# The order of TensorE's work within a step of an attention stage: weighing the values ahead of preparing later heads

## The chip, the cores and the metric

One core of a Trainium2 chip. The time is device microseconds (us) of one execution of the whole program. An engine is TensorE (PE; its weight loads are PEld), VectorE (DVE), ScalarE (ACT), GpSimd (POOL) or SyncE (SP, which here only issues DMAs).

## The reference

Attention over 2 batches, 8 heads, 768 positions and 64 columns, in which a query sees only keys of its own cluster (16 a head, the nearest centroid by cosine). Two feed-forward blocks over 1536 tokens follow.

```python
q_assign = np.argmax(np.einsum('bhsd,hcd->bhsc', q_n, c_n), axis=-1)
k_assign = np.argmax(np.einsum('bhsd,hcd->bhsc', k_n, c_n), axis=-1)
mask = q_assign[:, :, :, None] == k_assign[:, :, None, :]
scores = np.where(mask, scale * np.matmul(q, k.transpose(0, 1, 3, 2)), -1000000000.0)
scores = scores - np.max(scores, axis=-1, keepdims=True)
attn = np.exp(scores); attn = attn / (np.sum(attn, axis=-1, keepdims=True) + 1e-09)
x = heads side by side of np.matmul(attn, v)          # 1536 x 512
h = (x @ moe_w1) * (x @ moe_w2) @ moe_w3 @ moe_w_out
h = h @ moe2_w_in; out = (max(h, 0) + alpha * min(h, 0)) @ moe2_w_out
```

## The kernel before, in words

Every fp32 product is made from a rounded high part and a low remainder (names ending in h and l), as two or three fp32r matmuls. The order of work of all engines is written out by hand, step by step, and each engine has its own queue; they meet in semaphores.

The attention stage walks over the 16 heads in steps, one per tile of 128 queries (6 a head, 96 in all). A turn is 4 heads (24 steps): the first 11 steps are a prologue, then a loop and two written-out turns follow. In step c, TensorE's `step` (L667) puts into its queue:

- `score(c)` (L612): four matmuls into one of two PSUM slots. It waits until ScalarE's exponential has read tile c - 2.
- `turn_probabilities(c - 4)` (L631): six transposes of exponentials, three into each bank of `turned_p`, each bank once VectorE has read the low part `pl` of the tile before from it.
- what `prepared` (L54) lists for this step. It repeats every 12 steps: in steps 10, 11, 0 and 1 of the twelve half a head is turned (`turned`, L583: three transposes of q and k side by side into bank 0 of `acc`), in steps 2 and 3 a half of the cluster scores of two heads is made (`cluster`, L598: six matmuls into the same bank). All of these belong to heads that are scored later. Each waits until the bank is read (`prep_free`).
- `weigh(c - 5)` (L649): four matmuls that multiply turned probabilities by v and add them up in bank 1 of `acc` over three tiles. The first of a group of three (c = 2, 5, 8, 11 of the twelve) waits until ScalarE has copied the group before out of the bank (`drained`); the first tile of a head (c = 5 and 11) also waits for GpSimd's splitting of v (`v_done`).

ScalarE's `step` (L932): `out_copy` of a finished group (L921), the two copies `ph` of the turned probabilities (L914), scaling of the turned operands if there are any (`operands_hi`, L899), the exponential of tile c (L906), x's high part (`x_hi`, L927). In steps 2, 5, 8 and 11 the output copy comes first, and in steps 4 and 10 the high part last.

VectorE's `step` (L1163): the maximum of tile c (L1147), `pl` (L1152), then the low part of the operands (`operands_lo`, L1115), or the transposing of the cluster scores (L1123), or a step of picking the clusters (L1132).

GpSimd's `step` (L536): picking (L478), folding and normalising a finished head (L512), splitting v (L465), x's low part (L528). SyncE's `step` (L343) issues the DMAs for it: half a head of x moved to other partitions, copies of the operands that stack high and low parts (`stack_first` L300 behind a turned head, `stack_second` L307 behind the cluster scores), masks, the row of inverses, the next q, k and v.

The last turn prepares nothing. There are 26 turned tiles in steps (steps 0 and 1, then 24) and 14 halves of cluster scores (steps 2 and 3, then 12); the first ones stand in steps c = 0 to 3, where nothing is yet weighed. Behind the attention stage, from about 304 us, the feed-forward blocks run on the same engines.

Of the kernel before, what the change touches and what calls it, by code (L numbers as in the profile page):

```python
# [39 lines left out]
LT, LW, LX = 4, 5, 6  # L40
# [13 lines left out]
def prepared(it, c, last):  # L54

    j, m = c // 12 * 2, c % 12
    plan = {0: [("turned", j + 3, 0)], 1: [("turned", j + 3, 1)], 2: [("cluster", j + 2, 0)], 3: [("cluster", j + 2, 1)],
            4: [("pick1", j + 2, 0)], 6: [("pick2", j + 2, 0)], 9: [("pick3", j + 2, 0)],
            10: [("turned", j + 4, 0)], 11: [("turned", j + 4, 1)]}.get(m, [])
    there = HB if last else 2 * HB if isinstance(it, int) and it == TURNS - 2 else 3 * HB  # L60
    return [(kind, head, half) for kind, head, half in plan if head < there]
# [31 lines left out]
def build(nc, q, k, v, cen, w1, w2, w3, wo, w_in, w_out, alpha, out):  # L93
    ctx = ExitStack()
    with ctx:
# [162 lines left out]
        def tile(it, c):  # L258

            return TILES * it + c  # L260

        def head(it, j):

            return HB * it + j
# [313 lines left out]
        def _(pe):  # L578
            def mm(o, a, b, start, stop):
                return nc.tensor.matmul(o, a, b, start=start, stop=stop)  # L580


            def turned(it, j, half, first=False):  # L583

                f = fill_of(it, "turned", j, half)
                o = acc[:, half if first else 0, :]
                pe.wait_ge(ld_qk[j % 2], 32 * (2 * it + (j // 2 + 1)))
                if not first:
                    pe.wait_ge(prep_free, f)
                elif j > 0:  # L590
                    pe.wait_ge(prep_free, f - 1)
                for t in range(3):
                    last = nc.tensor.transpose(o[:, t * P:(t + 1) * P],
                                               qk[j % 2][:, 3 * half + t, :, :].rearrange("p a d -> p (a d)"),
                                               ident[:, :])
                last.then_inc(prep_full, 1)

            def cluster(it, j, half, first=False):  # L598

                f = fill_of(it, "cluster", j, half)  # L600
                cols, o = slice(half * HS, (half + 1) * HS), acc[:, half if first else 0, 0:HS]
                pe.wait_ge(prep_free, fill_of(it, "cluster", j, 0) if first else f)
                pe.wait_ge(cwin_done, head(it, j + 2))
                for e in range(2):
                    h = (j + e) % HB
                    w = cwin[h][:, :, 64 - 64 * e:192 - 64 * e]
                    mm(o, w[:, 0, :], q1[h][:, cols], e == 0, False)
                    mm(o, w[:, 1, :], q1[h][:, cols], False, False)
                    last = mm(o, w[:, 0, :], k1[h][:, cols], False, e == 1)
                last.then_inc(prep_full, 1)  # L610

            def score(it, c):  # L612


                j, t = divmod(c, T6)
                h, q_tile, o = j % HB, slice(t * P, (t + 1) * P), scores[c % 2]
                if c >= 2:
                    pe.wait_ge(exp_done, tile(it, c - 1))
                elif c == 1:
                    pe.wait_ge(w3_lo, NF)  # L620
                if t == 0:
                    pe.wait_ge(stacked2[h], 32 * (it + (j // HB + 1)))
                    pe.wait_ge(masked[h], 32 * (it + (j // HB + 1)))
                for half in range(2):
                    mm(o[:, half, 0:HS], q1[h][:, q_tile], k1[h][:, half * HS:(half + 1) * HS], True, False)
                for half in range(2):
                    last = mm(o[:, half, 0:HS], q2[h][0:96, q_tile], k2[h][0:96, half * HS:(half + 1) * HS],
                              False, True)
                last.then_inc(score_full, 1)

            def turn_probabilities(it, g):  # L631


                first_tile, a = g // 3 * 3, g % 3
                if a == 0:
                    pe.wait_ge(exp_done, tile(it, first_tile + 3))
                if g == 0:
                    pe.wait_ge(wc_out, NF)
                for b in range(2):
                    if g >= 1:  # L640
                        pe.wait_ge(pl_done, 2 * tile(it, g) + b - 1)
                    key_tile = 2 * a + b
                    for i in range(3):
                        p = pf[(first_tile + i) % NPF][:, :, :].rearrange("p a t -> p (a t)")
                        last = nc.tensor.transpose(turned_p[:, b, i * P:(i + 1) * P],  # L645
                                                   p[:, key_tile * P:(key_tile + 1) * P], ident[:, :])
                    last.then_inc(t_full, 1)

            def weigh(it, g):  # L649


                j, a = g // T6, g % 3
                pe.wait_ge(pl_done, 2 * tile(it, g) + 2)
                if a == 0:
                    if g == 0:
                        pe.wait_ge(prep_free, FILLS + 2)
                    else:
                        pe.wait_ge(drained, 2 * HB * it + g // 3)
                if g % T6 == 0:
                    pe.wait_ge(v_done, head(it, j + 1))  # L660
                for b in range(2):
                    w = v12[j % 2][:, 2 * a + b, :]
                    mm(out_acc, w, ph[g % NPH][:, b, :], a == 0 and b == 0, False)
                    last = mm(out_acc, w, pl[g % NPH][:, b, :], False, a == 2 and b == 1)
                last.then_inc(pv_done, 1)

            def step(it, c, last):  # L667
                there = lambda g: g >= 0 and (not last or g < TILES)
                if there(c):
                    score(it, c)  # L670
                if there(c - LT):
                    turn_probabilities(it, c - LT)
                for kind, j, half in prepared(it, c, last):
                    if kind == "turned":
                        turned(it, j, half)
                    elif kind == "cluster":
                        cluster(it, j, half)
                if there(c - LW):
                    weigh(it, c - LW)


            def turn_w3(f, parity):
# [74 lines left out]
            for c in range(LEAD):  # L757
                step(0, c, False)
                if c < 4:
                    if c % 2 == 0:  # L760
                        pe.wait_ge(wc_out, NF - 3 + c // 2)
                    product_wc(c // 2, range(4 * (c % 2), 4 * (c % 2) + 4))
            with pe.Fori(0, TURNS - 2) as it:
                for c in steps():
                    step(it, c, False)
            for c in steps():
                step(TURNS - 2, c, False)
# [545 lines left out]
```

## Time and profile before

| | |
|---|---|
| time, median of 3 runs | 787.78 us (786.77 to 788.28) |
| the profiled execution's time | 788.31 us |
| its span, first to last instruction | 786.5 us |
| mean granted TensorE clock | 0.993 of full speed |
| busy: TensorE, its weight loads | 762.0 us, 647.5 us |
| busy: VectorE, ScalarE, GpSimd | 418.9, 329.3, 188.1 us |
| attention stage | from about 56 to 304 us |

A row of the profile's groups and of the timeline names the line, the engine, the operation and what it writes and reads. Matmuls overlap, so TensorE's busy time says little about its peak; where a step stands is best read from the start of its weight loads. An idle time is given in brackets with what ended it.

### The profile page before, as it was taken

The numbers are of one execution on the slowest core, as the hardware profiler recorded it, in microseconds if no ns is written. First come the engines' busy times: TensorE is split into PE (matmuls) and PEld (weight loads), VectorE is DVE, ScalarE is ACT, GpSimd is POOL, SyncE is SP. The second block draws the span as 40 slices with busy tenths as digits, with TensorE's granted clock in tenths as the row PEclk, the third lists the DMA queues.
The fourth block names the chain that finished last, engine by engine and source line by source line (L and its number), as shares of the span: only waits on it lengthen the run. The fifth ranks groups of instructions, "written<-read, shape, count | busy, mean of one in ns | idle before, by whom it ended". The sixth has DMA issues, their size and how long they took to land.

```text
span 786.5 us, 10717 instructions
## 1 busy us (share of the span) xinstructions
PE 762.0 (97%) x3810; PEld 647.5 (82%) x3810; DVE 418.9 (53%) x636; ACT 329.3 (42%) x643; POOL 188.1 (24%) x210
## 2 busy tenths in 40 slices
PE   5999999999999998899999999999999999999998
PEld 4888998898899897788888888878888888888886
DVE  5335988989889886443211143276333443333332
ACT  4335978878888885532211142242112101020102
POOL 2131486876876873300000000000000000000000
PEclk9999999999999998999999999999999999999999
DMA  9645455554564322230000021232000000010001
GB/s 295 161 121 127 87 125 132 134 137 114 123 151 106 92 47 74 73 108 1 0 1 1 0 81 54 80 93 69 0 1 23 32 1 1 1 53 1 1 0 54
DMA packets 63579, 54.17 MB, mean 69 GB/s; under 512 B 31264, under 2 KB 51760, under 8 KB 63536
## 3 DMA queue, kind: packets, MB, share of 16 engines
q1 hardware_dynamic: 63536, 53.59, 26.4%
q8 instruction: 28, 0.46, 0.2%
q14 instruction: 15, 0.12, 0.0%
HBM read 31.50 MB, written 3.19 MB: 44 GB/s over the span
## 4 chain that ended last, share of the span: by engine, by line
PE 76%; POOL 15%; issue 5%; DVE 2%; ACT 2%; DMA 1%; POOLq 0%; SPq 0%; ACTq 0%
PE slot L580 55%; PE acc L580 17%; POOL xf L525 3%; PE slot L645 3%; POOL xf L521 2%; POOL xl L531 2%; POOL v L474 1%; POOL oh L500 1%; POOL v L470 1%; POOL c L492 1%; PE slot L693 1%; POOL c L493 1%; POOL c L498 1%; POOL c L490 1%; DMA early<-in_moe_w_out 1%
## 5 line engine op out<-in xcount | busy, mean ns | idle before, releaser
L580 PE MATMUL slot<-xh,w 128*128 128x512 f32 x768 | 252.7, 395 | 0.0
L580 PEld LDWEIGHTS slot<-xh,w 128*128 128x128 f32 x768 | 144.3, 188 | 34.9
L580 PE MATMUL slot<-xl,w 128*128 128x512 f32 x384 | 151.8, 395 | 0.0
L1049 ACT CAST gh<-gf 128x512 fp32r<-128x512 f32 x48 | 29.8, 621 | 207.8 <-PE acc L580 190.4
L1155 DVE TENSOR_TENSOR pl<-slot,ph 128x384 fp32r<-128x384 f32 x192 | 97.7, 549 | 14.0 <-ACT ph L919 13.8
L1149 DVE TENSOR_REDUCE nm<-slot 128x1 f32<-128x768 f32 x96 | 91.2, 950 | 21.4 <-PE slot L580 21.0
L919 ACT CAST ph<-slot 128x384 fp32r<-128x384 f32 x192 | 83.6, 487 | 40.4 <-PE slot L645 39.6
L911 ACT ACTIVATE pf<-slot,nm 128x768 f32<-128x768 f32 x96 | 87.9, 915 | 8.7 <-DVE nm L1149 8.5
L580 PEld LDWEIGHTS slot<-xl,w 128*128 128x128 f32 x384 | 72.2, 188 | 17.2
L645 PE MATMUL slot<-ident,pf 128*128 128x128 f32 x576 | 81.9, 277 | 1.9 <-DVE pl L1155 1.6
L580 PE MATMUL slot<-k,q 96*128 96x384 f32 (+1 forms) x384 | 83.6, 339 | 0.0
L1281 DVE TENSOR_TENSOR gl<-gf,gh 128x512 fp32r<-128x512 f32 x48 | 33.2, 692 | 91.4 <-ACT gh L1049 91.4
L580 PE MATMUL acc<-ph,v 128*128 128x384 f32 x192 | 72.7, 379 | 9.3 <-POOL v L474 4.0
L645 PEld LDWEIGHTS slot<-ident,pf 128*128 128x128 f32 x576 | 68.1, 142 | 11.0 <-DVE pl L1155 7.0
L580 PEld LDWEIGHTS slot<-k,q 96*128 96x128 f32 (+1 forms) x384 | 68.5, 189 | 0.3
L1228 DVE TENSOR_TENSOR ab<-slot,asb 128x512 f32<-128x512 f32 x24 | 16.5, 689 | 93.5 <-ACT asb L991 93.5
L1274 DVE TENSOR_SCALAR neg<-slot,al 128x512 f32<-128x512 f32 x48 | 36.0, 750 | 55.2 <-PE slot L580 55.2
L580 PE MATMUL acc<-pl,v 128*128 128x384 f32 x192 | 65.4, 341 | 0.0
L580 PE MATMUL slot<-w,gh 128*128 128x512 f32 x192 | 59.9, 393 | 0.0
L580 PE MATMUL acc<-w,gh 128*128 128x512 f32 x192 | 59.1, 389 | 0.0
L991 ACT COPY asb<-slot 128x512 f32<-128x512 f32 x24 | 14.1, 587 | 103.2 <-PE slot L580 103.2
L580 PEld LDWEIGHTS acc<-ph,v 128*128 128x128 f32 x192 | 36.7, 191 | 13.9 <-issue 10.9
(117 smaller groups left out, 1084.5 us busy)
## 6 DMA issues: line engine op xcount, KB each, us to landing
stage<-in_moe_w SPq DMA_DIRECT2D x16, 256.0 KB, 3.2
stage<-in_moe_w_in SPq DMA_DIRECT2D x16, 256.0 KB, 2.7
stage<-in_moe_w_out SPq DMA_DIRECT2D x16, 256.0 KB, 3.0
stage<-in_moe_w SPq DMA_DIRECT2D x6, 512.0 KB, 4.2
qk<-in_q SPq DMA_DIRECT2D x16, 192.0 KB, 3.8
qk<-in_k SPq DMA_DIRECT2D x16, 192.0 KB, 4.2
vn<-in_v SPq DMA_DIRECT2D x16, 192.0 KB, 3.9
q<-k SPq DMA_DIRECT2D x16, 192.0 KB, 3.4
```

What stands on the lines that cost most here:

```text
L521: nc.gpsimd.tensor_tensor(x, x, o, ALU.add).then_inc(folded, 1)
L525: nc.gpsimd.tensor_tensor(x, x, inverse, ALU.mult).then_inc(norm_done, 1)
L580: return nc.tensor.matmul(o, a, b, start=start, stop=stop)
L645: last = nc.tensor.transpose(turned_p[:, b, i * P:(i + 1) * P], p[:, key_tile * P:(key_tile + 1) * P], ident[:, :])
L911: nc.scalar.activation(pf[c % NPF][:, :, :], wide(scores[c % 2]), ACT.Exp, bias=nm[:, c % 4:c % 4 + 1], accum_out=sm[j % 2][:, t:t + 1]).t ...
L919: copy(ph[g % NPH][:, b, :], turned_p[:, b, 0:HS]).then_inc(ph_done, 1)
L1049: copy(gh[j % 2][:, :], gf[j % 2][:, :]).then_inc(gh_done, 1)
L1149: nc.vector.tensor_reduce(nm[:, c % 4:c % 4 + 1], wide(scores[c % 2]), AX.XY, ALU.max, negate=True).then_inc(max_done, 1)
L1155: tt_(pl[g % NPH][:, b, :], turned_p[:, b, 0:HS], f32(ph[g % NPH][:, b, :]), ALU.subtract).then_inc(pl_done, 1)
L1228: tt_(ab[f % 2][:, :], bank[2 * (f % 2) + 1], asb[f % 2][:, :], ALU.mult).then_inc(ab_done, 1)
L1274: ts(neg[:, :], h, 0.0, al[:, j:j + 1], ALU.min, ALU.mult).then_inc(neg_done, 1)
L1281: tt_(gl[j % 2][:, :], gf[j % 2][:, :], f32(gh[j % 2][:, :]), ALU.subtract).then_inc(gl_done, 1)
```

## The change

In TensorE's `step` the weighing of tile c - 5 is put ahead of the turned operands or cluster scores of the later heads. Nothing else is changed: instructions, buffers and semaphores are the same, and so are the orders of the other engines.

```diff
                 if there(c - LT):
                     turn_probabilities(it, c - LT)
+                if there(c - LW):
+                    weigh(it, c - LW)
                 for kind, j, half in prepared(it, c, last):
                     if kind == "turned":
                         turned(it, j, half)
                     elif kind == "cluster":
                         cluster(it, j, half)
-                if there(c - LW):
-                    weigh(it, c - LW)
```

## Rows read from the trace of the kernel before

**Rows 1.** The page: busy us, share of the span and instructions of each engine.

```profile
PE 762.0 (97%) x3810; PEld 647.5 (82%) x3810; DVE 418.9 (53%) x636; ACT 329.3 (42%) x643; POOL 188.1 (24%) x210
```

**Rows 2.** Windows: stretch, length, busy us (x instructions) of each engine, clock, DMA share, GB/s.

```profile
116.30:126.77 10.47, 9.91 (x67) 8.97 (x66) 9.99 (x17) 10.05 (x22) 5.94 (x6) 1.00 0.55 122
...
208.79:219.34 10.55, 9.89 (x67) 8.98 (x66) 10.07 (x17) 9.99 (x21) 8.15 (x10) 1.00 0.52 122
```

**Rows 3.** The chain that ended last, 200 to 230 us: start, us, what.

```profile
211.76 1.01 POOL v L474
...
212.90 0.94 PE acc L580 x4
213.84 0.71 PE slot L580 x4
214.55 0.66 PE slot L645 x6
215.21 0.33 PE acc L593 x3
215.54 0.70 PE acc L580 x4
...
220.01 1.74 PE acc L580 x10
...
227.54 0.47 DVE cmx L1139
...
228.15 0.85 POOL c L490
```

**Rows 4.** The timeline of TensorE's weight loads: start, us, engine, line, tile.

```profile
208.79 0.36 PEld L593 LDWEIGHTS acc<-ident,qk 128*128 128x128 f32 x3
...
212.87 0.19 PEld L580 LDWEIGHTS acc<-ph,v 128*128 128x128 f32 x1 [0.81 <-issue]
...
213.51 0.72 PEld L580 LDWEIGHTS slot<-k,q 128*128 128x128 f32 x4
...
219.02 0.75 PEld L645 LDWEIGHTS slot<-ident,pf 128*128 128x128 f32 x6
...
219.74 0.30 PEld L580 LDWEIGHTS acc<-q,cwin 128*128 128x128 f32 x2
...
221.41 0.71 PEld L580 LDWEIGHTS slot<-k,q 128*128 128x128 f32 x4
```

**Rows 5.** The timeline of ScalarE in the same round.

```profile
210.22 0.90 ACT L911 ACTIVATE pf<-slot,nm 128x768 f32<-128x768 f32 x1 [0.16 <-DVE nm L1149]
...
211.24 0.83 ACT L930 CAST xh<-xf 64x768 f32 x1
...
212.09 0.48 ACT L925 COPY xf<-acc 128x384 f32<-128x384 f32 x1
...
213.36 0.58 ACT L903 ACTIVATE q<-acc,scl 128x384 fp32r<-128x384 f32 x1
...
213.84 0.89 ACT L911 ACTIVATE pf<-slot,nm 128x768 f32<-128x768 f32 x1
...
214.97 0.86 ACT L919 CAST ph<-slot 128x384 fp32r<-128x384 f32 x2
...
218.59 0.91 ACT L911 ACTIVATE pf<-slot,nm 128x768 f32<-128x768 f32 x1
...
219.47 0.50 ACT L925 COPY xf<-acc 128x384 f32<-128x384 f32 x1
...
222.88 0.86 ACT L919 CAST ph<-slot 128x384 fp32r<-128x384 f32 x2 [1.26 <-PE slot L645]
```

**Rows 6.** The timeline where a scaling waited for its turned tile (prologue).

```profile
60.11 0.42 PEld L593 LDWEIGHTS acc<-ident,qk 128*128 128x128 f32 x3
...
60.81 0.58 ACT L903 ACTIVATE q<-acc,scl 128x384 fp32r<-128x384 f32 x1 [0.53 <-PE acc L593]
```

**Rows 7.** Waits of TensorE over the span: who for whom, us, times, longest.

```profile
PE acc L580 <- POOL v L474: 4.0, 6, 1.1
```

## The prediction

> **What bounds the kernel now.** I read the busy shares first: TensorE is busy 97% of the span [rows 1], so any of its time that is put in or taken out counts at first sight. But the change touches only the attention stage, so I took that stage by windows. The reader is to see a *round* there: of every twelve score steps, four (10, 11, 0, 1) turn the operands of a later head and two (2, 3) make cluster scores. From the turned tile of step 10 into the transposes of step 2, 10.55 us, TensorE, VectorE and ScalarE are all nearly full (9.89, 10.07, 9.99 us) at a granted clock of 1.00, the 2.4 GHz level [rows 2]. An engine in such a stretch can't take a wait without handing it on. The round three before has the same figures within a tenth; between their starts (116.30 and 208.79) lie three rounds of 30.83 us [rows 2].
>
> Next the chain that ended last. It goes from the splitting of v on GpSimd (ends at 212.77) into the weighing of step 11, stays on TensorE without a gap through steps 0, 1, 2 and 3, then goes through VectorE's pick (227.54) back to GpSimd (228.15), whose work leads to the next v [rows 3]. So GpSimd's part begins when TensorE's part is over: what steps 11 to 3 lose on TensorE starts the next GpSimd part later, and nothing in the loop absorbs it.
>
> The same chain gives TensorE's prices: scores of a step 0.71 us, six probability transposes 0.66, three operand transposes 0.33, four weighing matmuls 0.70; ten (four of them weighing) 1.74, so the six of a cluster half 1.04 [rows 3].
>
> **The change, part by part.** Nothing is added or removed: in TensorE's queue the weighing of tile c - 5 goes ahead of the operand transposes (four steps a round) and of the cluster matmuls (two). There are six rounds: steps 10 and 11 of the prologue with the four that follow, then one per twelve steps, and none in the last turn. The steps c = 0 to 3 have nothing to weigh and cost nothing.
>
> *Weighing earlier, gain 0.* What it releases sooner is the output copy of ScalarE and the buffers of ph. The copy of step 2 stands behind the exponential of step 1 (218.59 to 219.47) [rows 5], not behind the weighing, so ScalarE's queue hides the gain. The operands of the weighing, pl of the tile before, were waited for by the transposes just issued.
>
> *The turned tile later, in ScalarE's queue.* Its order stays: output copy, two copies ph, the scaling of the turned tile, then the exponential. The scaling now waits 0.70 us more, and behind it wait the exponential, x's high part in step 10, and the next output copy and ph. From the first weight load of a turned tile to a scaling that truly waited for it is 0.70 us (60.11 to 60.81) [rows 6]. Scaling to exponential is 0.48 (213.36 to 213.84), exponential to the next PSUM reader 0.88 (218.59 to 219.47), to x's high part 1.02 (210.22 to 211.24), that to the output copy 0.85 (to 212.09) [rows 5]. I walk one round with these; times are the trace's own.
>
> Step 10: the turned tile began at 208.79 [rows 4]; with 0.70 of weighing ahead it begins at 209.49 and is ready at 210.19. Exponential 210.67 (was 210.22), x's high part 211.69, output copy 212.54 to 213.02.
>
> Step 11: the weighing starts a new group, so it needs that copy as well as v. It started 0.13 behind v's end [rows 3]; 0.13 behind the copy is 213.15, where it was 212.87, having idled 0.81 [rows 4]. Today the turned tile sits under that idle time for nothing; moved behind, it costs its 0.33. Weighing took 0.64 (212.87 to 213.51) [rows 4]: turned tile 213.79, scores of step 0 at 214.12, where they were at 213.51. **Lost so far 0.61.**
>
> ScalarE: the tile of step 11 is ready at 214.49, exponential 214.97 (was 213.84), ph of step 0 at 215.85 (was 214.97) [rows 5]. TensorE runs step 0 from 214.12 in its 2.40 us: transposes 214.83, weighing 215.49, turned tile 216.19, ready 216.89. Exponential 217.37, ph of step 1 at 218.25. Step 1 from 216.52: turned tile 218.59, ready 219.29, exponential 219.77, output copy 220.65 to 221.15 (length 0.50 [rows 5]).
>
> Step 2 from 218.92: scores, transposes from 219.63, done issuing at 220.29. Its weighing starts a new group and needs that copy: 221.28. In the old order the cluster matmuls (219.74 [rows 4]) stood under it. With the cover gone TensorE idles 0.99 (the clock didn't fall over the 0.81 of step 11 [rows 2, 4]; I take none). Then 0.70 and 1.04: scores of step 3 at 223.02, where they were at 221.41 [rows 4]. **Lost in the round 1.61 us**, of which 0.61 was there before and 1.00 comes here.
>
> Behind that ScalarE had 1.26 us idle at 222.88 [rows 5], so its lag ends and is not carried on.
>
> *Cluster matmuls later.* Each of the two gives VectorE its tile 0.70 later. Its transpose needs to be done before the scores of the next step (0.71 later) give it a maximum: hidden, 0; with no cover it would cost at most that 0.70, put into the upper end.
>
> *VectorE.* In the four turned steps it has 0.48 us free in 10.55 [rows 2], and its k waits for the scaling, with the next maximum behind it. It starts about level with the lag; I take 0. Bounds: below 0, above 0.4 a round, most of what it has free, if its pl is then late for the next transposes.
>
> *DMA queue.* SyncE issues two copies behind each turned head, later by up to 1.2 us with the scaling, and four behind the cluster half of step 3, later by 0.70. Behind them stand a half of x, the row of inverses and the next v. The heads stacked there are scored nine steps on; x's half is folded by GpSimd in step 7, when its own chain is busy: 0. Uncovered, they would delay v of step 11 by the same 0.7 at most.
>
> Sum: 6 x 1.61 = 9.7 us. The profiled execution took 788.31 (span 786.5), so 798.0 of the same kind; the median of the runs is 787.78, half a microsecond lower, and gives **797.5 us**. From no change, a measurement of this kernel can tell about 0.2% (1.6 us).
>
> At the 0.70 rests much of it. The nearest other way is to take only the three transposes and their way through: the last starts 0.22 behind the first (0.33 by three) [rows 3]. "TensorE: Matmul & The Clock Gate" of the Trainium skill, section Single matmul latency, has (398 + N) / 2.4 ns at the 2.4 GHz level, 0.22 us for 128 columns. By that page the tile would be ready at 0.44 and not 0.70; no fp32 transpose stands in it, and the measured row is kept.
>
> **The rivals.**
> (a) *The turned tile is ready sooner than 0.70.* The row is from the start of the kernel, one of the few scalings that truly waited; its load spacing may be the start's. If two steps of the walk (10 and 1, the two whose readiness sets an output copy) gain 0.25 each, a round loses 1.11: 6.7 us, 794.4. For it: every later row in the attention has ScalarE busy, so the readiness isn't seen there. Against: the only row that shows it.
> (b) *Only the cover of step 11 is lost.* If ScalarE has room that I don't see, its lag is gone by step 2 and the clusters' cover wasn't needed: 0.61 a round, 3.7 us, 791.5. Against: ScalarE is 9.99 of 10.55 busy [rows 2] and its copy ended at 219.97, already behind the transposes' 219.68 (219.02 and 0.66) [rows 4, 5]. It decides if that copy ends by 220.16, 0.2 later than now; the walk has it 1.2 later.
> (c) *Not slower: v comes too early to matter.* The 4.0 us in six waits for v [rows 7] are GpSimd's. If GpSimd ran on its own clock round after round, a TensorE later by 1.6 would only meet v that waits for it less, and the loss would be taken from those waits: 787.8. It decides if GpSimd's chain doesn't start from TensorE. Against: it goes through VectorE's pick behind the scores of step 4 [rows 3], so v moves with TensorE.
> (d) *VectorE becomes the bound too.* At 10.07 of 10.55 it is the fullest [rows 2]; 0.4 a round more, 12.1 us, 799.9.
>
> **How the numbers follow.** Forecast 0.50; (a) 0.18; (b) 0.12; (c) 0.07; (d) 0.13. The predicted time is the forecast's. The range reaches down to (b), 791.3, and up to (d) with a little of the clusters' bound, 800.5; outside are (c) and misjudged sizes. Faster by over 0.2% has 0.03 and within 0.2% 0.06, shared from (c) and from a (b) smaller than worked out; slower 0.91.
>
> **What would show it.** In the changed profile: the scores of step 0 begin some 0.6 us later behind v; the first weighing matmul of step 2 idles about 1 us with ScalarE's copy of the accumulator as releaser, six times; ScalarE waits for the turned tile before its scaling, which it hardly does now; a round is 32.4 us instead of 30.8; the clock stays at 1.00 there; everything behind the last round is moved as a whole. Wrong would be: no wait for the copy in step 2 (b), waits for v gone and the round as long as before (c), or transposes that wait for pl in steps 1 and 2 (d).

## The result and the profile after

The changed kernel takes **796.42 us** (median of 4 runs, 794.37 to 797.91) beside 787.27 (786.77 to 788.28) of the kernel before in the same session: ratio 1.0113, 95% interval 1.0084 to 1.0142. The forecast was 797.5. The profiled execution took 797.46, its span is 795.7 and its mean clock 0.991.

The page of the changed kernel: busy times, the shares of the chain that ended last, and the group of weighing matmuls (TensorE's *weighing* is the four matmuls by v; *the copy* is ScalarE's reading of their accumulator, L925).

```profile
PE 763.4 (96%) x3810; PEld 647.6 (81%) x3810; DVE 419.8 (53%) x636; ACT 329.3 (41%) x643; POOL 188.0 (24%) x210
...
PE 89%; ACT 4%; issue 3%; POOL 2%; DVE 1%; DMA 0%; ACTq 0%; POOLq 0%; DVEq 0%
...
L580 PE MATMUL acc<-ph,v 128*128 128x384 f32 x192 | 73.8, 384 | 17.3 <-ACT xf L925 13.3
```

The same work takes the same busy time [rows 1]; 1.4 us more on TensorE is little beside 9.2 more in the span. So the loss is waiting. The chain that ended last is made differently, too; the same line of the kernel before:

```profile
PE 76%; POOL 15%; issue 5%; DVE 2%; ACT 2%; DMA 1%; POOLq 0%; SPq 0%; ACTq 0%
```

GpSimd, with 15% before, has 2% now, and ScalarE 4% instead of 2. The idle time ahead of the weighing is now ended mostly by ScalarE's copy of the accumulator, 13.3 of 17.3 us; before it was 9.3 us, with v as main releaser, 4.0 [rows 7]. The waits of TensorE over the whole span show the exchange:

```profile
PE acc L580 <- ACT xf L925: 13.3, 16, 1.4
...
PE acc L580 <- POOL v L474: 1.1, 1, 1.1
```

Of the 16 waits for the copy, four (2.4 us) stand in the kernel before as well, in step 5; six in step 11 and six in step 2 are new.

The windows of the changed kernel: the two stretches that answer to [rows 2], and three whole rounds from the scaling of a step 10 to the same one three rounds on (columns as there).

```profile
118.58:129.57 10.99, 9.63 (x66) 8.75 (x65) 9.48 (x16) 9.34 (x21) 6.46 (x6) 1.00 0.53 119
...
215.21:226.20 10.99, 9.67 (x67) 8.82 (x66) 9.55 (x17) 9.40 (x21) 7.15 (x9) 1.00 0.54 112
...
119.92:216.55 96.63, 89.08 (x578) 82.63 (x577) 82.79 (x143) 78.24 (x175) 68.10 (x68) 1.00 0.58 123
```

And the same three rounds of the kernel before:

```profile
116.98:209.47 92.49, 88.97 (x578) 83.04 (x577) 82.58 (x142) 78.34 (x175) 68.11 (x68) 1.00 0.56 128
```

Every engine is as busy as before, the clock is 1.00 in both, and only the length differs: a round is 96.63 / 3 = 32.21 us instead of 30.83, **1.38 more**, and six rounds make 8.3. That is the whole of it inside the attention: from the scaling of step 1 in the prologue to the end of the last exponential (where the reading of its sum starts) it is 243.96 us before (60.81 to 304.77) and 252.16 after (61.77 to 313.93), 8.2 more. Behind that exponential both take the same (481.7 and 481.8 us). The remaining 0.96 us of the profiled pair lies ahead of the attention, in code that the change doesn't touch; the start of the first scaling moves by such an amount from one execution to another in all kernels below (49.9 to 51.6 us). From here on kernels are therefore compared by the round, and by the median times.

The timeline of the changed kernel in the round walked through in the prediction; the times of the walk are 6.42 us earlier (transposes of step 10: 208.51 before, 214.93 after).

```profile
215.85 0.42 PEld L593 LDWEIGHTS acc<-ident,qk 128*128 128x128 f32 x3
...
216.55 0.58 ACT L903 ACTIVATE q<-acc,scl 128x384 fp32r<-128x384 f32 x1 [0.55 <-PE acc L593]
217.03 0.89 ACT L911 ACTIVATE pf<-slot,nm 128x768 f32<-128x768 f32 x1
...
218.18 1.00 POOL L474 TENSOR_TENSOR v<-vn,v 128x384 fp32r<-128x384 f32 x1
...
218.89 0.48 ACT L925 COPY xf<-acc 128x384 f32<-128x384 f32 x1
...
219.44 0.19 PEld L580 LDWEIGHTS acc<-ph,v 128*128 128x128 f32 x1 [1.53 <-issue]
219.47 0.41 PE L580 MATMUL acc<-ph,v 128*128 128x384 f32 x1 [1.32 <-ACT xf L925]
...
220.07 0.42 PEld L593 LDWEIGHTS acc<-ident,qk 128*128 128x128 f32 x3
...
220.46 0.65 PEld L580 LDWEIGHTS slot<-k,q 128*128 128x128 f32 x4
...
220.77 0.58 ACT L903 ACTIVATE q<-acc,scl 128x384 fp32r<-128x384 f32 x1 [0.64 <-PE acc L593]
...
224.85 0.42 PEld L593 LDWEIGHTS acc<-ident,qk 128*128 128x128 f32 x3
...
225.55 0.58 ACT L903 ACTIVATE q<-acc,scl 128x384 fp32r<-128x384 f32 x1 [0.18 <-PE acc L593]
...
226.90 0.48 ACT L925 COPY xf<-acc 128x384 f32<-128x384 f32 x1
...
227.49 0.19 PEld L580 LDWEIGHTS acc<-ph,v 128*128 128x128 f32 x1 [0.87 <-issue]
...
229.18 0.71 PEld L580 LDWEIGHTS slot<-k,q 128*128 128x128 f32 x4
```

The rows can be followed as a chain. In step 11 the weighing is held by ScalarE's copy (ends 219.37), no longer by v. But v ends only 0.19 sooner (219.18), so an earlier copy alone could win back 0.2 us there; TensorE's weight loads of the same place are in part still put down to v (4.8 us in three waits). The turned tile no longer lies under that wait but behind the weighing. The scaling waits for it, the exponential, ph and in step 1 the next copy (226.90) come later, and in step 2 the weighing is held by that copy for 0.87 us, where the cluster matmuls used to run [rows 4].

### The profile page after: what moved, and what is told of

Read it like the earlier page. It is cut to its first block, busy times and chain, and to the rows that moved or that the text cites. A ratio compares the mean times of both kernels' runs of the same rounds, so it can differ in the third digit from the quotient of the medians.

```text
span 795.7 us, 10717 instructions
## 1 busy us (share of the span) xinstructions
PE 763.4 (96%) x3810; PEld 647.6 (81%) x3810; DVE 419.8 (53%) x636; ACT 329.3 (41%) x643; POOL 188.0 (24%) x210
## 4 chain that ended last, share of the span: by engine, by line
PE 89%; ACT 4%; issue 3%; POOL 2%; DVE 1%; DMA 0%; ACTq 0%; POOLq 0%; DVEq 0%
PE slot L580 58%; PE acc L580 23%; PE slot L645 6%; PE acc L593 1%; ACT pf L911 1%; ACT xf L925 1%; PE slot L693 1%; ACT xh L930 1%; ACT ph L919 0%; DVE w L1214 0%; POOL xf L525 0%; DVE pl L1155 0%; ACT xh L891 0%; DMA cn<-in_centroids 0%; ACT w L980 0%
## 5 line engine op out<-in xcount | busy, mean ns | idle before, releaser
L1149 DVE TENSOR_REDUCE nm<-slot 128x1 f32<-128x768 f32 x96 | 90.8, 946 | 14.3 <-PE slot L580 13.1
L580 PE MATMUL acc<-ph,v 128*128 128x384 f32 x192 | 73.8, 384 | 17.3 <-ACT xf L925 13.3
L580 PE MATMUL slot<-k,q 96*128 96x384 f32 (+1 forms) x384 | 85.3, 343 | 0.0
L580 PEld LDWEIGHTS slot<-k,q 96*128 96x128 f32 (+1 forms) x384 | 66.9, 189 | 0.3
```

Of the source, the lines that this page charges most:

```text
L1149: nc.vector.tensor_reduce(nm[:, c % 4:c % 4 + 1], wide(scores[c % 2]), AX.XY, ALU.max, negate=True).then_inc(max_done, 1)
```

## The experiments

Two causes were forecast: the cover of step 11 and the cover of step 2 with ScalarE's lag between. Rivals: the turned tiles alone, the cluster halves alone, VectorE, v. The *round* is measured as above, in one trace of each kernel: a third of the distance between one scaling and the same three rounds on. All ratios are to the kernel before, which ran beside each (medians of 786.49 to 787.27 us); medians of different kernels are best compared by these ratios.

### One half of the change at a time

```diff
+                weigh_first = c % 12 in (2, 3)
+                if weigh_first and there(c - LW):
+                    weigh(it, c - LW)
                 for kind, j, half in prepared(it, c, last):
...
-                if there(c - LW):
+                if not weigh_first and there(c - LW):
```

This is the difference from the kernel before; the four kernels differ from each other only in the tuple: (2, 3), the cluster steps; (10, 11, 0, 1), the turned steps; (0, 1, 2, 3); and (10, 11).

> Weighing ahead of the cluster matmuls only (steps 2 and 3); the turned tiles stay ahead of it. A round of twelve steps (distance of the scalings three rounds apart, divided by three) is 30.83 us before and 32.21 after the change. Theory A (a wait for ScalarE's output copy in step 2, which is late because the turned tiles came late): here ScalarE isn't late, its copy ends at 219.97 by the trace of before and the transposes at 219.68, so the weighing of step 2 idles about 0.35 us and a round takes 31.15: 1.9 us over six rounds, about 789.2. Rival B (the lost cover of the clusters costs the same whether the turned tiles moved or not): the whole 0.84 of step 2, a round of 31.67, about 792.3.

> Weighing ahead of the turned tiles only (steps 10, 11, 0, 1); the cluster matmuls stay ahead of it. Theory A: step 11 loses the tile that stood under the wait for v and gets the later output copy (0.53 us from the transposes of step 10 to the scores of step 0 by the traces of before and after), and in step 2 the six cluster matmuls (1.05 us) again cover ScalarE's lag of 0.87, so nothing is lost there: a round of 31.36, 3.2 us over six rounds, about 790.5. Rival B (ScalarE's lag costs TensorE by itself, through the exponential or ph): a round near 32.2, about 795.5 with 8.2 us in all.

> Weighing first in steps 0 to 3 only; in steps 10 and 11 the turned tile is ahead of it as before. Theory A: the copy of step 2 hangs on the turned tile of step 1 alone, however early or late steps 10 and 11 ran, so step 2 has its whole loss and step 11 none: a round of 31.67 (0.84 more), 5.0 us over six rounds, about 792.3. Rival C (the lag builds up over all four turned tiles): half of it is gone without the first two, a round of about 31.3, 790.5.

> Weighing first in steps 10 and 11 only. Theory A: only the loss of step 11 is left (the turned tile that stood under the wait for v, and the copy of the accumulator that ends later), 0.53 us from the transposes of step 10 to the scores of step 0; ScalarE's lag is carried into steps 0 to 2 but its copy stands under the cluster matmuls there: a round of 31.36, 3.2 us in all, about 790. Together with the run on steps 0 to 3 (31.64 measured) the two parts then add up to the whole change (32.21). Rival C (the lag from step 11 makes steps 0 to 2 dearer too): a round of 31.7 or more.

| weighing first in | median us | ratio, 95% | round | more than 30.83 |
|---|---|---|---|---|
| 2, 3 | 788.61 | 1.0025, 1.0012 to 1.0038 | 31.05 | 0.22 |
| 10, 11, 0, 1 | 791.01 | 1.0044, 1.0030 to 1.0058 | 31.71 | 0.88 |
| 0, 1, 2, 3 | 791.28 | 1.0056, 1.0042 to 1.0071 | 31.64 | 0.81 |
| 10, 11 | 791.78 | 1.0062, 1.0041 to 1.0082 | 31.62 | 0.79 |
| all six | 796.42 | 1.0113, 1.0084 to 1.0142 | 32.21 | 1.38 |

Step 2 in the timeline of the kernel with only the cluster steps changed:

```profile
221.36 0.50 ACT L928 COPY xf<-acc 128x384 f32<-128x384 f32 x1
...
221.98 0.19 PEld L580 LDWEIGHTS acc<-ph,v 128*128 128x128 f32 x1 [0.32 <-issue]
```

And with steps 0 to 3 changed:

```profile
223.83 0.48 ACT L928 COPY xf<-acc 128x384 f32<-128x384 f32 x1
...
224.42 0.19 PEld L580 LDWEIGHTS acc<-ph,v 128*128 128x128 f32 x1 [0.87 <-issue]
```

Taking the cover away alone costs 0.32 at the weighing. With turned tiles moved in steps 0 and 1 as well the wait is 0.87, as in the full change, though steps 10 and 11 are as before. So ScalarE's lag in step 2 is set by the turned tile just before (step 1); step 11's part has caught up by then.

The parts don't add up: 0.22 + 0.88 = 1.10 is under 1.38, 0.79 + 0.81 = 1.60 above it. Where each kernel loses can be read from TensorE's weight loads, if the round is cut in two: from the weighing of step 11 to the scores of step 3, and from there to the next weighing of step 11, a stretch at whose end TensorE waits for v or the copy. One round of each, from about 151 us (the last kernel follows further down):

| weighing first in | step 11 to step 3, us | more | step 3 to step 11, us | more |
|---|---|---|---|---|
| none (before) | 8.52 | | 22.30 | |
| 2, 3 | 8.79 | 0.27 | 22.25 | -0.05 |
| 10, 11, 0, 1 | 9.15 | 0.63 | 22.56 | 0.26 |
| 0, 1, 2, 3 | 9.36 | 0.84 | 22.29 | -0.01 |
| 10, 11 | 9.05 | 0.53 | 22.58 | 0.28 |
| all six | 9.70 | 1.18 | 22.50 | 0.20 |
| all six, copy earlier | 8.86 | 0.34 | 22.29 | -0.01 |

The second stretch grows only where the turned tiles of steps 10 and 11 moved and the copy is late: there the copy comes behind v. In the first stretch a turned tile that no longer lies under the wait of step 11 is worth 0.39 (220.07 to 220.46 above). So the 1.38 of the full change are, by these rows, 0.39 for that tile, 0.20 for the copy in step 11, and 0.79 in step 2.

Both turned-only variants lose about 0.3 more than expected. For 0.12 of it the expectation was too low: it took 0.53 for steps 10 and 11 from the round at 208 to 221 us, and from the scores of step 10 to those of step 0 the three rounds before it lose 0.65 (7.02 instead of 6.37). The rest goes with a wait for VectorE's k, which still reads the turned tile: step 2 takes 3.33 instead of 3.10 in one of them, step 0 takes 2.51 instead of 2.40 in the other. The kernel before has such a wait in step 11 only (0.2 to 0.3), under the longer wait for v, and the changed one none: its weighing always lies between a turned tile and the next tile. Where the mixed orders switch, no weighing lies between, and the wait stands open. With the turned steps moved, in step 2:

```profile
224.07 0.62 DVE L1122 SCALAR_TENSOR_TENSOR k<-acc,scl,q 128x384 fp32r<-128x384 f32 x1
...
224.74 0.30 PEld L580 LDWEIGHTS acc<-q,cwin 128*128 128x128 f32 x2 [0.21 <-DVE k L1122]
```

With steps 10 and 11 moved, in step 0:

```profile
218.74 0.62 DVE L1122 SCALAR_TENSOR_TENSOR k<-acc,scl,q 128x384 fp32r<-128x384 f32 x1 [0.58 <-ACT q L906]
...
219.47 0.31 PEld L593 LDWEIGHTS acc<-ident,qk 128*128 128x128 f32 x3 [0.27 <-issue]
```

k ends at 224.69 and 219.36, the tile starts 0.05 and 0.11 behind it. Undoing half a change can thus add a wait of its own.

### ScalarE's queue: the exponential, or the copy, ahead of the scaling

The full change, with the exponential ahead of the scaling:

```diff
+                if there(c):
+                    probabilities(it, c)
...
-                if there(c):
-                    probabilities(it, c)
```

> The changed order on TensorE, and on ScalarE the exponential ahead of the scaling of the turned tile, so that ScalarE doesn't stand still with the exponential queued behind a tile that isn't there. Theory A: ScalarE works on the exponential while the turned tile comes, then scales, and its copy of step 2 ends near 219.97 by the clock of before and not 0.87 later: the loss of step 2 shrinks from 0.84 to about 0.35, that of step 11 stays near 0.5: a round of about 31.65, 5 us in all, about 792.3. Rival B (the lost cover alone, no matter what stands in ScalarE's queue): the round stays at 32.21, about 795.5.

Missed: 800.67 us, ratio 1.0181 (1.0164 to 1.0197), round 33.27, 1.06 longer than that of the full change where 0.56 less was expected. The timeline of that kernel:

```profile
229.72 0.62 DVE L1119 SCALAR_TENSOR_TENSOR k<-acc,scl,q 128x384 fp32r<-128x384 f32 x1 [0.61 <-ACT q L903]
...
231.24 0.90 ACT L911 ACTIVATE pf<-slot,nm 128x768 f32<-128x768 f32 x1 [0.80 <-DVE nm L1149]
```

The exponential needs the maximum, which stands behind k on VectorE, and k needs the scaling, now behind the exponential of the step before. The two queues wait for each other in turn, 14.3 us in 27 waits for nm and 16.0 in 23 for the scaling between 80 and 265 us.

The full change, with the copy of the accumulator one step earlier, behind ph:

```diff
-                out_head, half = drained_now(c, last)
+                if there(c - LT):
+                    probabilities_hi(it, c - LT)
+                out_head, half = drained_now(c + 1, last)
                 if out_head is not None:
                     out_copy(it, out_head, half)
-                if there(c - LT):
-                    probabilities_hi(it, c - LT)
```

> The changed order on TensorE, and on ScalarE the copy of the accumulator done a step earlier, right behind the copies ph, where ScalarE now waits for the turned tile. Theory A (the wait in step 2 is for that copy, which stands behind the turned tile's scaling and an exponential): by the trace of the changed kernel the copy then ends near 225.8 and not at 227.4, the weighing of step 2 follows the transposes at 226.5 instead of 227.5, and in step 11 the weighing waits for v alone: a round of about 31.1 instead of 32.21, 1.7 us in all over the kernel before, about 788.5. Rival (ScalarE is the engine that is full, wherever its copy stands): the time comes back as a later exponential or ph, a round of 31.6 or more, 791.5 or more.

The round is 31.10, as expected; the wait in step 2 is gone and v ends the wait in step 11:

```profile
214.52 0.19 PEld L580 LDWEIGHTS acc<-ph,v 128*128 128x128 f32 x1 [1.39 <-issue]
214.55 0.41 PE L580 MATMUL acc<-ph,v 128*128 128x384 f32 x1 [1.18 <-POOL v L474]
...
220.32 0.51 ACT L925 COPY xf<-acc 128x384 f32<-128x384 f32 x1
...
220.96 0.75 PEld L645 LDWEIGHTS slot<-ident,pf 128*128 128x128 f32 x6
...
221.68 0.19 PEld L580 LDWEIGHTS acc<-ph,v 128*128 128x128 f32 x1
```

But the time is 792.06 (ratio 1.0062, 1.0046 to 1.0078) and not 788.5. Behind the last exponential it takes 485.0 us instead of 481.7: TensorE waits 6.5 us at one place for VectorE's abl, the low part of the product of the first two feed-forward matmuls, where it was 2.0. The two rows, of this kernel and of the one before:

```profile
PE slot L580 <- DVE abl L1232: 6.5, 1, 6.5
...
PE slot L580 <- DVE abl L1232: 2.0, 1, 2.0
```

With the copies at the end of the last turn (c over 23) left in their old step that is gone too. The difference from the run above:

```diff
-                out_head, half = drained_now(c + 1, last)
+                out_head, half = drained_now(c if last and c > 23 else c + 1, last)
```

> The run with the copy of the accumulator behind ph, mended: the last two copies of the last turn keep their old place, since there the earlier copy stood in front of the work for the feed-forward block (TensorE waited 6.5 us for its first operand, 2.0 before). Theory A: the round stays at 31.10 and what follows the last exponential takes as long as before the change again: 1.6 us over the kernel before, about 788.7. Rival: the lost time behind the attention is the early copy's in the whole last turn, and the time stays at 791 to 792.

787.3 us, ratio 1.0007 (0.9998 to 1.0016), round 31.13. So an earlier copy takes back 1.08 of the 1.38: 0.84 between step 11 and step 3, and 0.21 where v now ends the wait (last row of the table above). The 0.30 that are left are in step 11, whose weighing still waits for v with no turned tile under the wait. In the median they don't show: six rounds of 0.30 would be 1.8 us, and the interval allows 1.3. The old order with only the copy moved was not run, so this run doesn't tell what the order itself costs once the copy is early.

### The wait for v

The kernel before with v split six steps earlier, into four buffers (one buffer each of ph and pl given up for the room):

```diff
-NPF, NPH = T6, 4
+NPF, NPH = T6, 3
...
-                if t == 2 and (not last or j < HB):
-                    split_v(it, j)
+                if t == 2 and (not last or j + 1 < HB):
+                    split_v(it, j + 1)
```

> The order of before, with v of each head split six steps earlier (four buffers for v's parts, three for ph and pl in return). Theory A: the wait for v in step 11 is GpSimd's alone, but ScalarE's copy of the accumulator ends only 0.2 us before v does, so the weighing of step 11 starts at most 0.2 earlier: a round of 30.6, 1.3 us less in all, about 785.5. Rival (GpSimd is the bound of the round and v its only hand over): the whole 0.8 us of idle time of step 11 goes, a round of 30.0, about 782.

785.42 us, ratio 0.9982 (0.9972 to 0.9992), round 30.73. The time is the one expected, but the round gains 0.10 and not 0.23; the rest of the 1.4 us lies outside the rounds compared, and where is not shown. The wait for v is gone, but the copy is hardly earlier than v was:

```profile
212.19 0.48 ACT L928 COPY xf<-acc 128x384 f32<-128x384 f32 x1
...
212.74 0.19 PEld L583 LDWEIGHTS acc<-ph,v 128*128 128x128 f32 x1 [0.58 <-issue]
```

The wait of 0.81 [rows 4] became one of 0.58. Both releasers have to move. The next two have early v and the early copy; they differ from each other only in TensorE's order, the changed one in the first, that of the kernel before in the second.

> The same with v split six steps earlier. Theory A: in step 11 of the run with the early copy TensorE idles 1.2 to 1.4 us for v alone; with v there, the weighing follows the transposes, the turned tile of step 11 is ready 0.9 sooner than ScalarE can take it, and ScalarE's queue sets the pace: a round of 30.2, 0.6 under the kernel before, 3.8 us less in all, about 783.5. Rival (VectorE and ScalarE are full): not more than the 0.1 a round that the earlier v gave in the old order (785.4).

> The same early copy and early v, with TensorE's order of before: the weighing last. It tells what the changed order is worth once the copy doesn't stand behind the turned tile. Theory A: the copy right behind ph then waits for a weighing that comes 0.33 to 1.05 later, with the scaling and the exponential behind it (0.8 later in step 10, 1.1 in step 1): a round of 30.9 to 31.2, 787 to 789, so that the changed order wins by 0.7 us or more a round. Rival (the order of TensorE doesn't matter once v is early): the same as the changed order within 1 us.

| TensorE's order | median us | ratio, 95% | round |
|---|---|---|---|
| weighing first | 781.36 | 0.9941, 0.9927 to 0.9954 | 30.36 |
| weighing last | 789.51 | 1.0037, 1.0023 to 1.0050 | 31.69 |

**The sign turns.** With v and the copy earlier the changed order is worth 1.33 us a round, 8.2 us in all, and gives a kernel 0.6% faster than the one before. Both differ from their expectations: the first was faster (783.5 expected, though its round of 30.36 is a little over 30.2), the second slower (a round of 30.9 to 31.2 and 787 to 789 expected). About half of the 8.2 is what the early copy costs the old order (ratio 1.0037 against 0.9982 with early v alone); against the old order at its best here, early v alone, the gain is 0.4%, about 3 us. In the old order the early copy waits on ScalarE for the weighing, 7.9 us in 20 waits; here is such a copy in the timeline of that kernel:

```profile
223.56 0.48 ACT L928 COPY xf<-acc 128x384 f32<-128x384 f32 x1 [0.44 <-PE acc L583]
```

And steps 1 and 2 in the timeline of the faster one, where neither engine waits:

```profile
217.00 0.51 ACT L928 COPY xf<-acc 128x384 f32<-128x384 f32 x1
...
217.63 0.75 PEld L648 LDWEIGHTS slot<-ident,pf 128*128 128x128 f32 x6
...
218.36 0.19 PEld L583 LDWEIGHTS acc<-ph,v 128*128 128x128 f32 x1
```

So the weighing first has a gain, the accumulator being done sooner, which the prediction costed at 0. Where the copy stands behind the exponential of the step before, as in the changed kernel, nothing of it is seen; the changed order with early v and the copy in its old step was not run.

What TensorE waits for in the faster kernel, from the view of waits between 80 and 262 us:

```profile
PEld slot L648 <- DVE pl L1158: 12.7, 40, 0.7
```

And its three rounds by windows:

```profile
118.30:209.37 91.07, 88.97 (x578) 81.82 (x577) 82.22 (x143) 78.69 (x176) 68.11 (x68) 1.00 0.58 130
```

The transposes wait 40 times for VectorE's pl (17 times, 3.4 us, over the same stretch of the kernel before), and VectorE is busy 82.22 of the 91.07 us; in the kernel before it was 82.58 of 92.49. It isn't VectorE alone: the longest wait of a round, 0.7, and one of 0.5 come where pl itself waited for ScalarE's ph (7.3 us in 15 waits), which there stands behind x's high part. The one in step 11:

```profile
210.86 0.83 ACT L933 CAST xh<-xf 64x768 f32 x1
...
212.23 1.02 DVE L1158 TENSOR_TENSOR pl<-slot,ph 128x384 fp32r<-128x384 f32 x2 [0.54 <-ACT ph L922]
...
212.84 0.31 PEld L648 LDWEIGHTS slot<-ident,pf 128*128 128x128 f32 x3 [0.53 <-DVE pl L1158]
```

### Turned tiles in other steps

The kernel before with early v, the copy right behind the exponential a step earlier, and the turned halves of head j + 4 in steps 8 and 9:

```diff
-            4: [("pick1", j + 2, 0)], 6: [("pick2", j + 2, 0)], 9: [("pick3", j + 2, 0)],
-            10: [("turned", j + 4, 0)], 11: [("turned", j + 4, 1)]}.get(m, [])
+            4: [("pick1", j + 2, 0)], 6: [("pick2", j + 2, 0)], 8: [("turned", j + 4, 0)], 9: [("turned", j + 4, 1), ("pick3", j + 2, 0)]}.get(m, [])
...
```

> The order of before, with v split earlier, the accumulator's copy ahead of x's high part on ScalarE, and the turned tiles of steps 10 and 11 moved to steps 8 and 9, where ScalarE has idle time. Theory A (steps 10 to 2 are bound by ScalarE and VectorE together, 9.99 and 10.07 of 10.55 us, behind a wait for v): two scalings (0.48 each) and two low parts (0.6 each) leave that stretch and no wait is left in step 11, so TensorE runs through at its own 28.3 us plus what steps 3 to 9 idle now (0.6 in step 5, 0.25 in step 8): a round of 29.3 to 29.8, six rounds 6 to 9 us less than before, about 779 to 781. Rival (GpSimd's chain bounds the round by itself): the round stays above 30.5 and the time within 2 us of before.

Missed: 800.97 us, ratio 1.0198 (1.0165 to 1.0231), round 32.22. The rounds make 8.3 of the loss, and another 3.0 lie behind the last exponential, as in the first run with the copy moved. The tile is asked for before its q and k have arrived from the DMA, 2.0 us in every round:

```profile
212.72 0.31 PEld L595 LDWEIGHTS acc<-ident,qk 128*128 128x128 f32 x3 [2.01 <-issue]
212.73 0.55 PE L595 MATMUL acc<-ident,qk 128*128 128x128 f32 x3 [1.78 <-DMA qk<-in_k]
```

The last one is the faster kernel with those halves in steps 7 and 8, and the loads of q and k issued from step 1 on:

```diff
-                if c % 12 in (5, 7) and c // 12 * 2 + 4 + c % 12 // 7 in loads:
+                if c % 12 in (1, 7) and c // 12 * 2 + 4 + c % 12 // 7 in loads:
```

> The kernel with the changed order, early copy and early v, and the turned tiles of steps 10 and 11 in steps 7 and 8, with the load of their q and k issued four steps earlier (the run that moved them to 8 and 9 had TensorE waiting 2.0 us for that load). Theory A: the loss of that run was the load alone; steps 10 to 2 lose two scalings and two low parts, a round of 29.6 to 30.0, bounded by VectorE's 29.5 us of work: 1 to 4 us under the run without the move, 780 to 783. Rival (VectorE, with the pick of step 9 close by, is pushed back there instead): no gain, or a loss of up to 1 us.

782.75 us, ratio 0.9953 (0.9939 to 0.9967), round 30.32: no gain over 30.36, where 29.6 to 30.0 was expected, so this is a miss too, and its rival (no gain) is what came. The wait for the load is gone. Its three rounds have VectorE busy 81.66 of 90.95 us, and TensorE's wait for pl stays (13.0 us in 40). Moving those scalings moves nothing while TensorE waits for pl; whether VectorE's own queue or ScalarE's ph holds pl was not separated.

## Why the prediction was right

The time (forecast 797.5, measured 796.42) and the place were right. Its walk against the changed timeline:

| | walk + 6.42 | measured |
|---|---|---|
| turned tile, step 10 | 215.91 | 215.85 |
| scaling, exponential | 216.61, 217.09 | 216.55, 217.03 |
| copy, step 11 | 218.96 | 218.89 |
| weighing, step 11 | 219.57 | 219.44 |
| scores, step 0 | 220.54 | 220.46 |
| turned tile, step 1 | 225.01 | 224.85 |
| copy, step 2 | 227.07 | 226.90 |
| weighing, step 2 | 227.70 | 227.49 |
| scores, step 3 | 229.44 | 229.18 |

- **Step 11, 0.61 forecast:** scores of step 0 came 5.53 us behind the transposes of step 10, before 5.00: 0.53. In the three rounds before this one it is 0.65.
- **Step 2, 1.00 forecast:** the whole way to the scores of step 3 is 14.25 instead of 12.90, so 0.82 lie here (0.76 in the three rounds before); the weighing idled 0.87, forecast 0.99. That makes 1.35 in the walk, and 1.38 as a mean of three rounds.
- **The terms that were mis-sized,** 0.23 a round together: the weighing ahead of a turned tile was taken as 0.70 from the chain and is 0.64 from first load to next load (215.21 to 215.85), and it is in the chain twice; the hand-over from the copy to the weighing was taken as 0.13 from the row of v and is 0.07 (219.37 to 219.44) and 0.11 (227.38 to 227.49); the copy is 0.48 in step 2 and not 0.50; the weighing and the cluster half of step 2 take 1.69 to the next scores (227.49 to 229.18), not 1.74. The 0.13 was misread besides: it is the start of the matmul behind v (212.77 to 212.90), but was set against starts of weight loads, where v's is 0.10 (212.87). The other way, a turned tile between matmuls of the other type takes 0.39 to the next scores (220.07 to 220.46), not 0.33; those scores are then 0.64 long (220.46 to 221.10) and not 0.71.
- **Weighing earlier, gain 0:** true in this kernel, where the copy stands behind an exponential. It is no property of the order, as the pair of kernels with the early copy shows.
- **From 8.3 to 9.2:** six rounds account for 8.3 of the 9.15 between the medians; the rest lies within what the parts outside the attention differ by from run to run (last section). Against the 9.15 the forecast's 9.7 is 0.5 too long, against the 8.3 of the mechanism 1.4: a part of the nearness is luck, from 0.85 us that the rounds don't explain.
- **Rival (a), turned tile ready sooner than 0.70:** rejected. The three scalings of the timeline above all waited, and each came 0.70 behind the first load (215.85 to 216.55, 220.07 to 220.77, 224.85 to 225.55). The Trainium skill ("TensorE: Matmul & The Clock Gate", Single matmul latency) has its formula for a single bf16 matmul. The prediction's estimate from it for three fp32 transposes, 0.44, doesn't agree with the trace; the measured 0.70 decides.
- **Rival (b), only step 11:** rejected, the wait in step 2 is there in every round. The lag of which it asked was set by the turned tile of step 1, as the kernel with steps 0 to 3 shows.
- **Rival (c), v absorbs it:** rejected. v did move with TensorE: it ends 5.71 us behind the scores of step 10 (213.47 to 219.18), before 5.70 (207.06 to 212.76). The wait that ends last was handed to the copy, by 0.19 us.
- **Rival (d), VectorE:** not in the changed kernel, where it has more room than before (9.48 of 10.99 us). In the faster kernel TensorE waits for its pl, but there ScalarE's ph has a share.
- Cluster tiles, the DMA queue and the clock, all taken as 0: nothing in the trace of the round contradicts it.

## What to carry to other kernels

Before moving work behind something in a full engine's queue, ask what wait it lay under, and follow it through the in-order queue of the engine that reads it until that queue next has idle time: the price appeared a step later, at a wait for another buffer. An order of one engine is right or wrong only together with the place where the reader stands: here the same swap cost 9 us with the copy behind the exponential, and saved 8 with the copy behind ph and v early (about 3 against the old order in the placement that suits it best among those run). And an experiment that undoes half a change needs its own look at the waits, since a mixed order can shorten the distance between two users of a buffer.

## What was not expected of the hardware

Behind the attention the kernels run the same instructions, and yet in the eight whose copies stand in their old step the time from the last exponential to the end is between 477.7 and 481.8 us. It goes with the granted clock in a few stretches there. Two windows of the kernel before, around the end of its last exponential (304.77):

```profile
300.00:304.00 4.00, 1.74 (x8) 1.37 (x9) 3.00 (x5) 3.10 (x7) 1.19 (x1) 0.82 0.44 131
...
304.00:308.00 4.00, 4.00 (x15) 3.81 (x15) 2.06 (x5) 2.87 (x5) 3.35 (x4) 0.50 0.11 25
```

And the same stretches of the program in the kernel with steps 0 to 3 moved, 5.46 us later:

```profile
305.46:309.46 4.00, 1.74 (x10) 1.27 (x10) 3.00 (x5) 3.09 (x7) 1.18 (x1) 1.00 0.44 131
...
309.46:313.46 4.00, 4.00 (x22) 3.24 (x21) 2.92 (x5) 2.68 (x5) 3.35 (x4) 1.00 0.11 25
```

0.50 is the 1.2 GHz level, 1.00 the 2.4 GHz one. TensorE was busy 1.74 of 4 us in the first window of both; in one the clock fell before its end and was 0.50 in the next, in the other it stayed. From 296 to 346 us the mean is 0.90 in the kernel before and in the changed one (481.7 and 481.8 us behind the exponential), 0.93 in three that took 479.9 to 480.0, 0.97 in one with 479.0, and 1.00 in two with 477.7, one of them shown here. It differs between executions of one kernel as well: the kernel before took 788.3 to 788.9 us where its mean clock over the run was 0.993 and 785.6 to 787.2 where it was 0.998. What decides it for an execution stays open. It is 1 to 4 us, as much as some of the effects above, and the reason why the round was used to compare.
